# Gated linear attention with two mixture layers: shorter routing chain, one-hot rows tile by tile, gate products one pair later, and the two row products of attention in the other order

## The reference, cut to what matters

```python
for t in range(S):                                   # attention, per head: q, k, v of 4 x 8 x 768 x 40
    m_new = max(f_gate[t] + m, i_gate[t])
    f_stab, i_stab = exp(f_gate[t] + m - m_new), exp(i_gate[t] - m_new)
    C = f_stab * C + i_stab * outer(v[t], k[t]);  n = f_stab * n + i_stab * k[t]
    y[t] = sigmoid(o_gate[t]) * (C @ q[t]) / max(abs(n @ q[t]), 1)
x = y as (3072 tokens, 320)
e = argmax(x @ w_gate, 8 experts)                    # routing, gate = exp(0) / sum(exp(logits - max))
x[token] = gate * (relu(x @ w1[e]) @ w2[e])          # 320 -> 1024 -> 320
out = max(0.01 * h, h) @ w_out,  h = x @ w_in        # 320 -> 2048 -> 320
```

## Time and profile before

| | |
|---|---|
| median of 3 runs (lowest to highest) | 835.92 us (832.53 to 836.61) |
| the profiled execution | 834.39 us, of which the span is 832.7 us |
| busy in the span | TensorE 746.0, VectorE 531.0, ScalarE 388.3, GpSimd 146.5 us |
| granted TensorE clock, mean | 0.976 of full speed |

### The profile page before, as it was taken

One profiled execution on the slowest core, in us unless ns is written; L12 is line 12 of the kernel. 1 busy time (PEld: TensorE's weight loads), 2 busy tenths in 40 slices (PEclk: granted clock), 3 DMA queues, 4 the chain that ended last, 5 costly groups with the idle time before them and its releaser, 6 DMA issues.

```text
span 832.7 us, 17702 instructions
## 1 busy us (share of the span) xinstructions
PE 746.0 (90%) x6435; PEld 552.7 (66%) x6436; DVE 531.0 (64%) x1382; ACT 388.3 (47%) x713; POOL 146.5 (18%) x202
## 2 busy tenths in 40 slices
PE   0798999898178899999999989999999999999994
PEld 0577888787157788887888855555555555555552
DVE  7468999898776656766476666555455465554441
ACT  2457464664625557545654323343343433433432
POOL 4334443344131111111010000020010100100101
PEclk9999999999589999999999999999999999999998
DMA  9559999992052995397540000000000000000000
GB/s 235 150 151 307 296 298 288 275 282 83 9 150 95 327 348 198 125 357 271 190 152 2 2 2 2 1 32 1 1 33 1 24 8 0 31 0 1 32 2 31
DMA packets 49401, 99.75 MB, mean 120 GB/s; under 512 B 7822, under 2 KB 38222, under 8 KB 46766
## 3 DMA queue, kind: packets, MB, share of 16 engines
q1 hardware_dynamic: 39906, 67.65, 26.9%
q10 hardware_dynamic: 6780, 22.10, 7.8%
q0 software_dynamic: 2640, 9.01, 3.2%
HBM read 74.85 MB, written 23.89 MB: 119 GB/s over the span
## 4 chain that ended last, share of the span: by engine, by line
PE 81%; DMA 6%; DVE 5%; issue 3%; SPq 2%; ACT 1%; POOL 1%; ACTq 0%; DVEq 0%
PE bank L1524 33%; PE bank L1658 19%; PE bank L1558 12%; PE bank L1391 4%; PE bank L1420 3%; DMA vv<-v_in 2%; DMA d_parts<-xreg 1%; PE bank L1412 1%; PE bank L1514 1%; PE bank L1404 1%; PE bank L1443 1%; PE bank L1381 1%; PE bank L1383 1%; DMA d_x<-og 1%; PE bank L1635 1%
## 5 line engine op out<-in xcount | busy, mean ns | idle before, releaser
L1524 PE MATMUL bank<-stage,slot 128*128 128x512 f16 x768 | 181.1, 379 | 0.0
L1658 PE MATMUL bank<-slot,dec 128*128 128x320 f16 x768 | 159.1, 299 | 0.0
L1524 PE MATMUL bank<-qbd,slot 128*128 128x128 f16 x1984 | 120.1, 223 | 11.1 <-issue 11.1
L1524 PEld LDWEIGHTS bank<-qbd,slot 128*128 128x128 f16 x1984 | 116.2, 100 | 14.2 <-issue 13.9
L1524 PEld LDWEIGHTS bank<-stage,slot 128*128 128x128 f16 x768 | 75.1, 98 | 74.3 <-DVE stage L1323 0.2
L1327 DVE TENSOR_TENSOR qk<-stage,dec 128x512 f16<-128x512 f32 x96 | 66.4, 692 | 84.8 <-ACT dec L853 84.8
L1658 PE MATMUL bank<-slot,qk 128*128 128x320 f16 x384 | 114.8, 299 | 0.0
L1323 DVE TENSOR_TENSOR stage<-bank,stage 128x512 f32<-128x512 f32 x96 | 66.2, 690 | 67.4 <-ACT stage L847 66.9
L853 ACT CAST dec<-stage 128x512 f16<-128x512 f32 x96 | 59.4, 619 | 100.7 <-PE bank L1658 72.8
L1658 PEld LDWEIGHTS bank<-slot,dec 128*128 128x128 f16 x768 | 75.1, 98 | 44.3 <-DVE qk L1327 0.2
L1558 PE MATMUL bank<-slot,emov 128*128 128x320 f16 x496 | 102.0, 299 | 2.3 <-issue 1.5
(11 more groups left out here) (260 smaller groups left out, 1126.4 us busy)
## 6 DMA issues: line engine op xcount, KB each, us to landing
slot<-d_w SPq DMA_DIRECT2D x12, 1280.0 KB, 7.0
d_w<-slot ACTq DMA_DIRECT2D x4, 2560.0 KB, 8.9
stage<-wB SPq DMA_DIRECT2D x6, 1280.0 KB, 7.2
stage<-wA SPq DMA_DIRECT2D x6, 1024.0 KB
d_w<-slot SPq DMA_DIRECT2D x4, 1280.0 KB, 8.9
stage<-wB ACTq DMA_DIRECT2D x4, 1280.0 KB, 14.3
qk<-qkT SPq DMA_DIRECT2D x12, 360.0 KB
slot<-qkT SPq DMA_DIRECT2D x12, 360.0 KB
```

The source lines that it names most:

```text
L1524: ins = t_.matmul(pf, a[:, col:col + P], x(k), start=(q == 0), stop=(q == len(ops) - 1))
L1658: ins = t_.matmul(bank[4 + q][:, 0:DM], x[f % 2][:, q * P:(q + 1) * P], slotB[2 + f // NF][:, c0:c0 + DM], start=(f == 0 and z == 0), stop ...
```

## The change

In attention, `rows` multiplies the gates by the numerators first, as soon as `combine` is done, and by `den` second; the two semaphores that VectorE waits for are exchanged to match. In routing, the counts are read in PSUM by the three instructions that need them; the ones come from GpSimd; the exponentials' sum and its reciprocal move behind the index copy; `bid` has a semaphore of its own; and the 24 one-hot tiles are written by 24 instructions with a bf16 row of numbers and a per-partition scalar, TensorE waiting for each. In the expert layer the gate products stand behind the first product of pair 1, with `gates` moved on VectorE to match.

```diff
+        ones_r = q0[:, 4 * RN:5 * RN]
+        iota_b = q1[:, m1 + 8 * NE:m1 + 8 * NE + P // 2].bitcast(BF16)
...
             def rows(st, f, i):
+                pool.wait_ge(comb_done, NG * (st + 1))
+                pool.wait_ge(eo1_done, st + 1)
+                g.tensor_tensor(o3, num[i][:, :, 0:D], o3, ALU.mult).then_inc(bb_done, 1)
                 pool.wait_ge(den_done, st + 1)
-                pool.wait_ge(eo1_done, st + 1)
-                g.tensor_tensor(o3, o3, den[:, :].unsqueeze(2).broadcast_to([P, H, D]), ALU.mult).then_inc(bb_done, 1)
                 pool.wait_ge(bb_done, st + 1)
-                g.tensor_tensor(o3, num[i][:, :, 0:D], o3, ALU.mult).then_inc(x_done, 1)
+                g.tensor_tensor(o3, o3, den[:, :].unsqueeze(2).broadcast_to([P, H, D]), ALU.mult).then_inc(x_done, 1)
...
+            g.memset(ones_r, 1.0).then_inc(rt_const, 1)
+            g.iota(iota_b, pattern=[[1, P]], base=0, channel_multiplier=0,
+                   allow_small_or_imprecise_dtypes=True).then_inc(rt_const, 1)
...
             def combine(u, st, c, b, g, i, j, first=False):
                 if g == 0 and not first:
-                    dve.wait_ge(x_done, st - 1)
+                    dve.wait_ge(bb_done, st - 1)
...
             def denominator(st, j):
-                    dve.wait_ge(bb_done, st)
+                    dve.wait_ge(x_done, st)
...
-            rl(v.memset(c1[:, :, :], 1.0))
-            dve.wait_ge(rt_exp, 1)
-            rl(v.tensor_reduce(gw[:, :], lgs[:, :, :], AX.X, ALU.add))
-            rl(v.tensor_scalar(gw[:, :], gw[:, :], 1e-9, None, ALU.add))
-            rl(v.reciprocal(gw[:, :], gw[:, :]))
             dve.wait_ge(rt_cnt, 1)
-            rl(v.tensor_copy(r1, psS[1][:, 0:NE * NST]))
+            totals = psS[1][:, 0:RN]
-            rl(v.tensor_reduce(cnt, r1.rearrange("p (e t) -> p e t", e=NE), AX.X, ALU.add))
+            rl(v.tensor_reduce(cnt, totals.rearrange("p (e t) -> p e t", e=NE), AX.X, ALU.add))
...
-            rl(v.tensor_tensor_scan(cum, c1[:, :, :].rearrange("p t e -> p (t e)"), r1, 0.0,
-                                    ALU.mult, ALU.add))
+            rl(v.tensor_tensor_scan(cum, ones_r, totals, 0.0, ALU.mult, ALU.add))
...
-            rl(v.tensor_tensor(r1, cum, r1, ALU.subtract))
+            rl(v.tensor_tensor(r1, cum, totals, ALU.subtract))
...
-            rl(v.tensor_scalar(bid[:, :, 1, :], bid[:, :, 1, :], pcol[:, 0:1], None, ALU.mult))
-            for t0, t1 in ((0, 12), (12, NST - 1)):
-                tj = [P, t1 - t0, P]
-                v.tensor_tensor(oha[:, t0:t1, :], iota_j[:, :].unsqueeze(1).broadcast_to(tj),
-                                plo[:, t0:t1].unsqueeze(2).broadcast_to(tj), ALU.is_equal).then_inc(rt_a, 1)
-            v.tensor_tensor(ohl, iota_j[:, :], plo[:, NST - 1:NST].broadcast_to([P, P]), ALU.is_equal).then_inc(rt_a, 1)
+            v.tensor_scalar(bid[:, :, 1, :], bid[:, :, 1, :], pcol[:, 0:1], None, ALU.mult).then_inc(rt_bid, 1)
+            for t in range(NST):
+                v.tensor_scalar(onehot(t), iota_b, plo[:, t:t + 1], None, ALU.is_equal).then_inc(rt_a, 1)
...
             (behind the last use of `tke`, in the wait for the gather)
+            dve.wait_ge(rt_exp, 1)
+            rl(v.tensor_reduce(gw[:, :], lgs[:, :, :], AX.X, ALU.add))
+            rl(v.tensor_scalar(gw[:, :], gw[:, :], 1e-9, None, ALU.add))
+            rl(v.reciprocal(gw[:, :], gw[:, :]))
...
             (VectorE: `gates()` leaves the place ahead of x_low(2, 0) and stands in pair 1, behind jobs(1))
...
             (TensorE)
+            pe.wait_ge(rt_bid, 1)
             for t in range(NST):
-                pe.wait_ge(rt_a, 1 if t < 12 else 2 if t < NA else 3)
+                pe.wait_ge(rt_a, t + 1)
...
             h_product(0, 0, expert(0))
+            x_turn(2, 0)
+            h_product(1, 1, expert(1))
             pe.wait_ge(rt_bg, 3)
             for n_ in range(3):
                 for t in range(NST):
                     ins = t_.matmul(psT[:, n_ * NPAIR:(n_ + 1) * NPAIR], onehot(t), bg[n_][:, t, :],
                                     start=(t == 0), stop=(t == NST - 1))
             ins.then_inc(rt_gate, 1)
-            x_turn(2, 0)
-            pair(1, 1)
+            y_product(0, 0, expert(0))
+            x_turn(3, 1)
             pair(2, 0)
```

More of the change, by code:

```diff
@@ L186, in build @@
         rt_const = sem("rt_const")
+        rt_bid = sem("rt_bid")
         rt_exp, rt_oh, rt_cnt = sem("rt_exp"), sem("rt_oh"), sem("rt_cnt")
@@ L243, in build, with onehot @@
         ohl = dec[0][:, 0:P // 2].bitcast(BF16)
+        def onehot(t):
+            return oha[:, t, :] if t < NA else ohl
         bid = qk[0][:, :, :, :].rearrange("p n g t -> p (n g t)")[:, 0:NST * NPAIR].bitcast(BF16).rearrange("p (t v q) -> p t v q", t=NST, v=2)
@@ L582, in _ @@
             g.memset(trib, 1.0).then_inc(rt_const, 1)
+            g.memset(ones_r, 1.0).then_inc(rt_const, 1)
+            g.iota(iota_b, pattern=[[1, P]], base=0, channel_multiplier=0,
+                   allow_small_or_imprecise_dtypes=True).then_inc(rt_const, 1)
             g.iota(iota_e, pattern=[[1, NE], [0, NST]], base=0, channel_multiplier=0,
                    allow_small_or_imprecise_dtypes=True).then_inc(rt_const, 1)
-            pool.wait_ge(rt_const, 3)
+            pool.wait_ge(rt_const, 5)
             g.affine_select(out=trib, in_=trib, compare_op=ALU.is_gt, fill=0.0, base=0,
@@ L1085, in _ @@
             dve.wait_ge(lgc_done, NST)
-            dve.wait_ge(rt_const, 3)
+            dve.wait_ge(rt_const, 5)
             dve.wait_ge(late_done, LATE)
@@ L1256, in _ @@
             jobs(0)
-            gates()
             x_low(2, 0)
@@ L1266, in _ @@
                 jobs(p)
+                if p == 1:
+                    gates()
                 y_gate(p - 1)
@@ L1499, in _ @@
             logits(NST - 1)
-            pe.wait_ge(rt_const, 4)
+            pe.wait_ge(rt_const, 6)
             pe.wait_ge(rt_oh, 1)
@@ L1569, in expert @@
                 return pe.value_load(tab_exp[0:1, ds(p, 1)], min_val=0, max_val=NE - 1)
-            def onehot(t):
-                return oha[:, t, :] if t < NA else ohl
             pe.wait_ge(d_done, NST * NG)
+            pe.wait_ge(rt_bid, 1)
             for t in range(NST):
-                pe.wait_ge(rt_a, 1 if t < 12 else 2 if t < NA else 3)
+                pe.wait_ge(rt_a, t + 1)
                 for v_ in range(2):
@@ L1589, in _ @@
             h_product(0, 0, expert(0))
[L1590 to L1595, removed]
             x_turn(2, 0)
@@ L1607, in pair @@
                 x_turn(p + 2, i)
-            pair(1, 1)
+            h_product(1, 1, expert(1))
+            pe.wait_ge(rt_bg, 3)
+            for n_ in range(3):
+                for t in range(NST):
+                    ins = t_.matmul(psT[:, n_ * NPAIR:(n_ + 1) * NPAIR], onehot(t), bg[n_][:, t, :],
+                                    start=(t == 0), stop=(t == NST - 1))
+            ins.then_inc(rt_gate, 1)
+            y_product(0, 0, expert(0))
+            x_turn(3, 1)
             pair(2, 0)
```

## The result

The changed kernel takes 840.89 us (median of 5 runs, 840.23 to 843.83), the kernel before in the same session 835.11 us: a ratio of 1.0082 with a 95% interval of 1.0057 to 1.0106, slower by 0.8% (the ratio goes by all runs; that of the two medians, which lie 5.8 us apart, is 1.0069). The profiled execution took 842.22 us, its span is 840.5 us; before it was 834.39 and 832.7.

A forecast was written before the change was run, and what follows sets the result against it. TensorE's matmul stages set most of the time, VectorE's list most attention steps. 834.39 + 6.3 (attention) - 1.05 (routing with tail) - 1.0 (gate products) = 838.6 us, forecast as 839, range 831 to 844.

The forecast's parts named there:

- What bounds attention: Attention: VectorE and TensorE are full at once; in most steps VectorE's list sets the pace, each added microsecond lengthening the step.
- The hold: Attention: VectorE's small multiplication on `den` is held 0.43 us a step under GpSimd's early row product; 6.3 us slower in sum.
- the stretches of my sum: Attention's denominators by time: first four 0.3 us, ten to 134 us 4.0, three from 140 to 158 -0.6, six more 2.6.
- Tail: End of attention: the last transpose starts at about 210.3 us, set by the copy of the logits; 0.4 us saved.
- Routing: From the counts to the index copy: with the tail, 0.4 + 0.9 + 0.1 - 0.35 = 1.05 us faster.
- Counts: Routing: with the counts read in PSUM, four instructions and the copy ahead of L1107 go away; 0.90 us saved.
- the waits up to the one-hot rows: Routing: L1143 is no longer waited for, which gives 0.1 us.
- one-hot rows to the index copy: Routing: 24 instructions at 0.165 us plus 0.6 behind them, 4.56 us against 4.21; 0.35 us slower.
- The row taken for the price: Routing: L1306, 64 fp32 elements with a per-partition scalar, 0.16 us to its successor, prices each one-hot instruction.
- The gate products: Expert layer, first pairs: behind pair 1's first product no thin stretch slows it; 1.2 us saved, 1.0 taken.
- the bounds: Gate products: 0.3 us saved if the slow stretch only moves, 2.9 if the 1.68 us stall goes as well.
- the forecast's own case: Whole kernel: the forecast's terms hold, the small multiplication being held; 836 to 842 us, chance 0.45.

The follow-up runs named there:

- x5: The changed kernel without the multiplication of `den` by 2 (the ones forming the denominator are 2.0 instead): 836.22 us, ratio 1.0008 to the kernel before.
- x6: The kernel before with the changed routing and without the multiplication of `den`; old order of row products, gate products at their old place: 833.16 us, ratio 0.9971.
- x7: The changed kernel with thin loads, the weight loads of units 5 to 9 cut to a sixteenth of their columns: 835.45 us, one run.
- x10: x9 with the loads of unit 5 issued only behind pair 1's product: 834.81 us, ratio 0.9998 to the kernel before.
- x12: The changed kernel with thin loads for units 5 to 9 and the gate products at their old place: 833.62 us, one run.
- x4: The changed kernel with the gate products back at their old place, ahead of pair 1's product: 839.54 us, ratio 1.0041 to the kernel before.
- x8: The kernel before with the routing part of the change alone: 835.63 us, ratio 1.0006 to the kernel before.
- x9: x5 with the gate products at their old place: 833.12 us, ratio 0.9978 to the kernel before.

## Why the prediction was right in part

*What bounds attention.* Right, and x5 and x6 show the other side: both engines are at their limit, so a longer VectorE lengthens the steps and a shorter one gives next to nothing.

*The hold.* Right in kind and place; the size was 0.51 us and not 0.43. L1032 ends at 94.79 + 0.67 = 95.46, so with 0.17 us of its own it was let go at 95.29, which is 0.14 us before the product's end at 95.43 and not 0.21. I counted 20 of 24 steps in parts and got 6.3; the mean of the kernels is 6.1, the changed kernel's own 6.64. Of the 23 distances from reciprocal to reciprocal 19 grew, by 0.12 to 0.64 us, 8.76 in all; four got shorter, by 2.12, nearly all of it in three that a wait for a load had lengthened before. By the stretches of my sum: 0.89 ahead of 66 us (I had 0.3), +4.16 for the ten denominators up to 134 us (4.0), -1.09 for the three from 140 to 158 (-0.6), +2.56 for the six from 166 to 203 (2.6). So the count by stretches was good. What I had overlooked is the second hold, of 0.18 us in 8 steps, under `gate_one`. The section that I named, "Who interferes with whom" on the page "SBUF — State Buffer" of the Trainium skill, lists `tensor_scalar` among what can take the shared ports, and says that an instruction with at most one SBUF input, outside the two-port modes, does not contend; it does not name the reciprocal. The runs agree in kind: multiplication held (0.67), reciprocal free (0.20). They differ from "the whole instruction" in that the hold ended 0.14 us before the product's recorded end.

*The start.* 2.06 us of the 7.83 are the later first reciprocal. 0.5 of it is the first hold. The rest isn't the change's: over the thirteen kernels this instruction starts anywhere from 36.09 to 39.42 us, held or not.

*Tail.* -0.37 us (last combine to last transpose 2.27 us for 2.64), forecast -0.4; the profile has the transpose still waiting for the row product (L562), not for the copy that I had named. Behind it the last logits took 0.64 us less, with 0.91 us of matmuls in place of 1.53; this I had not seen coming.

*Routing.* Counts -0.91 (forecast -0.90), the waits up to the one-hot rows -0.12 (-0.1), one-hot rows to the index copy +0.27 (+0.35), starts 0.162 us apart (0.165), 0.55 us of the gather's wait left (0.5). The row taken for the price, a multiplication with a per-partition scalar on as many bytes, was the right one. The estimate by the Trainium skill's page "VectorE: DVE Perf Modes", section on the TRN2 errata, 0.094 us each, would have made the part 24 x 0.068 = 1.6 us too fast.

*The gate products.* The step that failed. I had written "In the new order the transpose for pair 2 and the product of pair 1 follow pair 0 without a thin stretch: 0.35 + 0.87 = 1.2 us saved", took 1.0, and allowed the 1.68 us stall to stay, go, or move with its matmuls. I took it as a property of the gate products. It goes with the load of unit 5 (x7, x10), and by the packets TensorE waits in it for code that comes late. It strikes 4.9 to 5.4 us behind the start of pair 0's product in either order: in the new order that is in pair 1's product, and a second one follows in the gate products. The stalls take 2.33 + 2.72 = 5.05 us in place of 1.68, 3.37 more; the rest of the stretch takes 14.50 us in place of 15.94, 1.44 less, near the 1.2 that I had. So the term that failed is the stall, which I left as it was in the forecast and let only disappear in the bounds. +1.93 us in the profiled execution, 1.2 on average. Without the loads the forecast's sign is right, 0.63 us (x12).

In sum the median rose by 5.8 us where I had 3.1, and if the average of the stretch reaches the end, the gate products are 2.2 us of the difference (-1.0 forecast, +1.2 on average). 840.9 lies within the 836 to 842 of the forecast's own case.

What stays open: when a packet starts was read from the traces and not varied by itself. x6's stall of 3.40 us, the longest first stall, goes with the latest packet, 5.56 us behind pair 0's product, but why that one is late no run tells. A second stop isn't peculiar to the new place: in x4, x8 and x9, with the gate products at the old one, TensorE stands another 1.7 to 2.3 us ahead of pair 0's second product, and its cause was not tried.

## What to carry to other kernels

Before starting GpSimd work earlier, list the VectorE instructions that would then lie under it and look for each one's kind: here 8 elements cost half a microsecond a step, while a reciprocal of the same size cost nothing. Folding the factor of 2 into a constant took the hold away, though it did not make this kernel faster than before. Where two engines are both full, price a change on the side where it lengthens, and expect little where it shortens. Read a stall of TensorE with no semaphore against the packets of the instruction queue and the loads beside it, and compare starts of the same instruction, not stalls: a stall that grows may only take the place of a slower product.

## What the hardware showed that I had not expected

As far as the packets tell, TensorE's code comes in pieces of 16 KB through the same engines as the loads. With the load queue at 91% of all sixteen engines a piece started 3.7 us later behind the same point of the code than with thin loads (5.13 against 1.47 us), and TensorE stood for 2.33 us; the next piece came when the load was through, and TensorE stood for 2.72 us beside nearly idle engines. With thin loads, or with the load moved away, it did not stand at all in this stretch. A stall of this kind ends some 2.5 us behind the start of its piece, and the one ahead of pair 4's product does so with any loads. The stall ahead of pair 3's product is 1.7 to 1.9 us in all thirteen kernels, with thin loads too, so that one has another cause than the loads.
